# Delta-rule attention in front of two expert stages: scores and changes on the far half of the partitions, outputs as one 128-row matmul per head

## What is computed

```python
# 1: delta rule, for each batch and head
k_n = k / (norm(k) + 1e-06)
for t in range(S):
    y[:, :, t] = q[:, :, t] @ state
    v_old = k_n[:, :, t] @ state
    state = state + beta[t] * outer(k_n[:, :, t], v[:, :, t] - v_old)
# 2: four experts on all tokens, weighted by normalised domain_probs
for e in range(4):
    out += p[:, e:e + 1] * (maximum(x @ w1[e], 0.0) @ w2[e])
# 3: eight experts, each token goes to its best one
logits = normalised(x) @ normalised(emb).T / tau
out[mask_e] = gate[mask_e, None] * (maximum(x[mask_e] @ w1[e], 0.0) @ w2[e])
```

## Time and profile before

| | us |
|---|---|
| median of 3 runs | 1420.02 (1417.57 to 1420.48) |
| the profiled execution | 1416.41 |
| its span | 1414.6 |
| TensorE busy in the span | 1315.2 |
| VectorE, ScalarE, POOL busy | 640.3, 471.1, 625.4 |

### The profile page before, as it was taken

The page is one execution under the profiler, slowest core; times in us unless marked ns, Lnnn a source line. Parts: engine busy times, 40 slices in busy tenths (PEclk is TensorE's granted clock), DMA queues, the critical chain, the costliest instruction groups (busy, mean ns, idle before and its releaser), DMA issues. The chain is left out here.

```text
span 1414.6 us, 31948 instructions
## 1 busy us (share of the span) xinstructions
PE 1315.2 (93%) x13279; PEld 1142.1 (81%) x13280; DVE 640.3 (45%) x1056; ACT 471.1 (33%) x794; POOL 625.4 (44%) x652
## 2 busy tenths in 40 slices
PE   5589999899999999999999999999995599999996
PEld 4468888788888888888788888887784599999996
DVE  7844544354453635437354262223623234636342
ACT  2223223433234422343233433334432213424231
POOL 3382248523684338823487235544652122222221
PEclk9599999999999999999999999999997699999998
DMA  6051233433434243342433323353442224525210
GB/s 237 2 210 58 76 103 103 152 96 65 120 100 172 83 79 109 115 162 72 96 109 97 93 64 84 110 197 108 97 134 75 71 86 129 167 89 172 92 31 23
DMA packets 66401, 149.91 MB, mean 106 GB/s; under 512 B 10676, under 2 KB 26481, under 8 KB 64744
## 3 DMA queue, kind: packets, MB, share of 16 engines
q1 hardware_dynamic: 53512, 116.66, 27.6%
q10 hardware_dynamic: 7776, 20.06, 4.5%
q0 software_dynamic: 4992, 11.44, 2.7%
HBM read 135.85 MB, written 11.48 MB: 104 GB/s over the span
## 5 line engine op out<-in xcount | busy, mean ns | idle before, releaser
L421 POOL TENSOR_TENSOR wsl<-raw,wsh 128x768 fp32r<-128x768 f32 x138 | 253.1, 1835 | 430.1 <-ACT wsh L544 429.8
L783 DVE SCALAR_TENSOR_TENSOR hl<-bank,hh 128x512 fp32r<-128x512 f32 x192 | 132.4, 690 | 498.8 <-ACT hh L548 485.9
L548 ACT ACTIVATE hh<-bank 128x512 fp32r<-128x512 f32 x192 | 114.7, 598 | 584.0 <-PE bank L1176 572.3
L1187 PE MATMUL bank<-hh,wsh 128*128 128x512 f32 x576 | 234.5, 407 | 5.2 <-DVE tmp L813 5.2
L1174 PE MATMUL bank<-xhl,wsh 128*128 128x512 f32 x576 | 225.9, 392 | 6.2 <-DMA xhl<-xhl 4.7
L1188 PE MATMUL bank<-hh,wsl 128*128 128x512 f32 x576 | 226.1, 392 | 0.0
L1189 PE MATMUL bank<-hl,wsh 128*128 128x512 f32 x576 | 225.6, 392 | 0.2 <-issue 0.2
L1175 PE MATMUL bank<-xhl,wsh 128*128 128x512 f32 x576 | 224.9, 390 | 0.0
L1176 PE MATMUL bank<-xhl,wsl 128*128 128x512 f32 x576 | 224.8, 390 | 0.0
L544 ACT ACTIVATE wsh<-raw 128x768 fp32r<-128x768 f32 x192 | 160.7, 838 | 7.8 <-DMA raw<-in_w_soft 7.7
L1174 PEld LDWEIGHTS bank<-xhl,wsh 128*128 128x128 f32 x576 | 108.8, 189 | 30.7 <-issue 4.8
(11 more groups left out here) (206 smaller groups left out, 2134.3 us busy)
## 6 DMA issues: line engine op xcount, KB each, us to landing
raw<-in_w_soft SPq DMA_DIRECT2D x192, 384.0 KB, 3.1
rawT<-in_w_top ACTq DMA_DIRECT2D x48, 384.0 KB, 3.7
kq<-in_kq SPq DMA_DIRECT2D x12, 1024.0 KB, 8.8
pb<-p_scratch SPq DMA_DIRECT2D x24, 256.0 KB, 3.8
rawT<-in_w_top SPq DMA_DIRECT2D x16, 384.0 KB, 6.5
kN<-in_kn SPq DMA_DIRECT2D x6, 768.0 KB, 4.8
vN<-in_vn SPq DMA_DIRECT2D x6, 768.0 KB, 5.4
xs_scratch<-xrow SPq DMA_DIRECT2D x20, 192.0 KB, 3.7
```

Of the source, the lines that this page charges most:

```text
L421: nc.gpsimd.tensor_tensor(wsl[:, n % WB, :], raw[:, n % RB, :], f32(wsh[:, n % WB, :]), ALU.subtract).then_inc(wlp_ok, 1)
L548: nc.scalar.activation(hh[:, n % 2, :], ps_h[n % 2][:, :], ACT.Relu).then_inc(hi_ok, 1)
L783: nc.vector.scalar_tensor_tensor(out=hl[:, n % 2, :], in0=ps_h[n % 2][:, :], scalar=0.0, in1=f32(hh[:, n % 2, :]), op0=ALU.max, op1=ALU.su ...
L1187: nc.tensor.matmul(o, wsh[:, w, cols], hh[:, n % 2, :], start=(f == 0), stop=False)
```

## The change

One tile `QP` now holds, for each head, q features on its own half of the partitions and the masked scores on the other ("far") half. One tile `SU` holds S and U of a head the same way; both are zero in the rows that belong to neither. The output of a head is one matmul over 128 partitions, SU against QP. To get there `scores` and `solved` write to the far half, `deltas` (ScalarE), `masked` and `state` (VectorE) work in two ops, one per head, and kN is stored with its halves exchanged; the squares of k are made from a load of their own, `ks`. q is no longer double-buffered: its two halves are loaded behind the v load. In a scan slot the order on TensorE is now solved, recalled, changes, outputs, the recall of the next step and the change of state of the last one each as a block. `scores` of chunk 0 are masked on VectorE after `back(0)`, no longer by POOL. The sums, norms, system and diagonal of chunk 1 stand behind the states of chunk 0 on VectorE, gram(1) right in front of the loop on TensorE, and the inverse of chunk 1 in slot 1 of POOL's loop. LATE becomes [9, 3, 0, 0, 0, 0].

The diff, cut; left out are the other wide blocks (the same edits as in the scan), renamed arguments and the arrays made on the host.

```diff
-        kq = sb(att, "kq", [P, 2, 2, NPAIR, NCH, HALF])
+        kT = sb(att, "kT", [P, 2, NPAIR, NCH, HALF])
...
-        PT = sb(att, "PT", [P, NU, HALF])
+        QP, SU = sb(att, "QP", [P, 2, NU, HALF]), sb(att, "SU", [P, 2, NPAIR, D])
...
-    ps_ks, ps_u = (bank_s[0][:, AL * D * i:AL * D * i + AL * D].rearrange("p (a d) -> p a d", a=AL) for i in range(2))
+    ps_u, ps_ds = (bank_s[0][:, AL * D * i:AL * D * i + AL * D].rearrange("p (a d) -> p a d", a=AL) for i in range(2))
     ps_yT = bank_s[1][:, 0:256].rearrange("p (a n) -> p a n", a=AL)
-    ps_ds = bank_s[1][:, 256:256 + AL * D].rearrange("p (a d) -> p a d", a=AL)
+    ps_ks = bank_s[1][:, 256:256 + AL * D].rearrange("p (a d) -> p a d", a=AL)
...
-    LATE = [3, 1, 0, 0, 0, 0]
-    INV_SLOT = 18
+    LATE = [9, 3, 0, 0, 0, 0]
+    INV_SLOT, FIRST_INV = 18, 1
     ROUTE = 3
     def att_slot(t, s):
     def inverting(m):
         begun = [SPT * t + INV_SLOT + LATE[t] for t in range(NT - 2)]
-        return m < 6 or any(b <= m < b + 12 for b in begun)
+        return FIRST_INV <= m < FIRST_INV + 12 or any(b <= m < b + 12 for b in begun)
...
+    def load_q(eng, c, hh2):
+        if c:
+            eng.wait_ge(ds_mm, UN * c)
+        eng.dma_start(QP[ROWS_T[hh2], hh2, :, :].rearrange("p u n -> p (u n)"), q_d[c, hh2]).then_inc(q_in, 16)
+
...
         sp.dma_start(en[:, :], emb).then_inc(e_in, 16)
         sp.dma_start(taub[:, 0:1], tau.partition_broadcast(P)).then_inc(e_in, 16)
+        load_squares(0)
+        sp.dma_start(beta[:, :, :], beta_d).then_inc(b_in, 16)
+        load_k(0)
+        load_q(sp, 0, 0)
+        load_v(0)
         load_kn(0)
-        sp.dma_start(beta[:, :, :], beta_d).then_inc(b_in, 16)
-        load_features(0, 0)
-        load_features(0, 1)
-        load_v(0)
-        load_features(1, 0)
-        load_kn(1)
+        load_k(1)
         for n in range(RB):
             load_raw(n)
+        load_squares(1)
+        load_kn(1)
         sp.dma_start(pr[:, :, :], probs_d).then_inc(p_in, 16)
-        load_features(1, 1)
...
         load_v(1)
+        for hh2 in range(2):
+            load_q(sp, 1, hh2)
...
             if s == 1 and t + 2 < NC:
                 load_kn(t + 2)
-                load_features(t + 2, 0)
-                load_features(t + 2, 1)
+                load_k(t + 2)
+                load_squares(t + 2)
             if a == 17 and t + 2 < NC:
                 load_v(t + 2)
+                for hh2 in range(2):
+                    load_q(sp, t + 2, hh2)
...
-        def mask_scores():
-            pool.wait_ge(pc_ok, VN)
-            nc.gpsimd.tensor_tensor(PT[:, :, :], PT[:, :, :], upper[:, :].unsqueeze(1).to_broadcast([P, NU, HALF]),
-                                    ALU.mult).then_inc(p_ok, VN)
-
...
         constants()
-        mask_scores()
         pool.wait_ge(inv_step, INV_STEPS)
         values(0)
         for n in range(2):
             low(n)
-        start_inverse(pool, nc.gpsimd, 1)
-        invert(pool, nc.gpsimd, 1)
-        values(1)
...
+            if n == FIRST_INV:
+                start_inverse(pool, nc.gpsimd, 1)
+                invert(pool, nc.gpsimd, 1)
+                values(1)
...
-            act.wait_ge(kn_in[c % 2], 16 * (c // 2 + 1))
-            if c:
-                act.wait_ge(ssq_ok, 2 * c)
-            nc.scalar.activation(sq[:, :, :], kN[:, c % 2, :, :], ACT.Square).then_inc(sq_ok, 1)
+            act.wait_ge(sq_in, 16 * (c + 1))
+            nc.scalar.activation(sq[:, :, :], sq[:, :, :], ACT.Square).then_inc(sq_ok, 1)
...
             m = UN * c + k
-            if k < UN - 1:
-                act.wait_ge(ks_mm, m + 2)
-            else:
-                act.wait_ge(u_mm, m + 1)
-            if m >= 2:
-                act.wait_ge(ds_mm, m - 1)
-            nc.scalar.activation(U[:, k % 2, :, :], ps_u, ACT.Copy).then_inc(u_ok, 1)
+            act.wait_ge(u_mm, m + 1)
+            act.wait_ge(ch_mm, m)
+            if m >= NB:
+                act.wait_ge(ds_mm, m - NB + 1)
+            pairs = slice(AL * (k % NB), AL * (k % NB) + AL)
+            for hh2, rows in enumerate(ROWS_FAR):
+                last = nc.scalar.activation(SU[rows, hh2, pairs, :], ps_u[rows], ACT.Copy)
+            last.then_inc(u_ok, 1)
         def x_high(c, k):
             ch, b, _ = units_of(k)
             cols = slice(P * b + HALF * ch, P * b + HALF * ch + HALF)
             act.wait_ge(ds_mm, UN * c + k + 1)
+            act.wait_ge(gks_ok, min(UN * c + k + 3, UN * c + UN))
...
+            if v == 0 and c == 0:
+                dve.wait_ge(mask_set, MASKS)
+            scores = score_banks[min(c, 1)][v]
+            for hh2, rows in enumerate(ROWS_FAR):
+                last = nc.vector.tensor_tensor(QP[rows, hh2, eight_pairs(v)[2], :], scores[rows],
+                                               upper[rows].unsqueeze(1).to_broadcast([HALF, 8, HALF]), ALU.mult)
+            last.then_inc(p_ok, 1)
...
             dve.wait_ge(ks_mm, m + 1)
-            if k:
-                dve.wait_ge(u_ok, m)
+            dve.wait_ge(ds_mm, m - 1)
...
-            if m >= NB:
-                dve.wait_ge(s_ok, m - NB + 1)
-            nc.vector.tensor_tensor(S[LIVE, pairs, :], S[LIVE, pairs, :], ps_ds[LIVE, :, :],
-                                    ALU.add).then_inc(s_ok, 1)
+            dve.wait_ge(u_ok, min(m + 2, UN * c + UN))
+            dve.wait_ge(s_ok, m - NB + 1)
+            for hh2, rows in enumerate(ROWS_D):
+                S = SU[rows, hh2, pairs, :]
+                last = nc.vector.tensor_tensor(S, S, ps_ds[rows], ALU.add)
+            last.then_inc(s_ok, 1)
...
         back(0)
-        sums(1)
-        norms(1)
         for v in range(VN):
-            system(1, v)
-        diagonal(1)
+            masked(0, v)
         for i in range(2):
             wide_first_state(i)
...
         for i in range(2):
             wide_state(i)
+        sums(1)
+        norms(1)
+        for v in range(VN):
+            system(1, v)
+        diagonal(1)
         probabilities()
...
-                    k, q = (kq[ROWS_D[hh2], c % 2, i, a0 + a, ch, :] for i in range(2))
-                    last = nc.tensor.matmul(dst[ROWS_T[hh2], a, :], k, q, start=True, stop=True)
+                    k, q = kT[ROWS_D[hh2], c % 2, a0 + a, ch, :], QP[ROWS_D[hh2], hh2, NPAIR * ch + a0 + a, :]
+                    last = nc.tensor.matmul(dst[ROWS_FAR[hh2], a, :], k, q, start=True, stop=True)
             last.then_inc(p_mm, 1)
...
+            pe.wait_ge(u_ok, m)
+            pe.wait_ge(s_ok, m - 1)
+            for al in range(AL):
+                for rows, far in zip(ROWS_T, ROWS_FAR):
+                    last = nc.tensor.matmul(ps_u[far, al, :], TT[rows, units.start + al, :], R[rows, k % 2, al, :],
+                                            start=True, stop=True)
+            last.then_inc(u_mm, 1)
+
+        def recalled_wait(c, k):
+            m = UN * c + k
+            if k == 0:
+                pe.wait_ge(p_ok, VN * (c + 1))
+            pe.wait_ge(s_ok, m - NB + 1)
+            pe.wait_ge(gks_ok, m)
+            pe.wait_ge(xl_ok, m - 2)
+
+        def changes_wait(c, k):
+            m = UN * c + k
+            if k == 0:
+                pe.wait_ge(kn_in[c % 2], 16 * (c // 2 + 1))
+            pe.wait_ge(u_ok, m + 1)
+            pe.wait_ge(xl_ok, m)
+            pe.wait_ge(s_ok, m)
+
+        def recalled(c, k, al):
+            ch, b, _ = units_of(k)
+            pair = AL * b + al
+            for hh2, rows in enumerate(ROWS_D):
+                last = nc.tensor.matmul(ps_ks[ROWS_T[hh2], al, :], kT[rows, c % 2, pair, ch, :], SU[rows, hh2, pair, :],
+                                        start=True, stop=True)
+            if al == AL - 1:
+                last.then_inc(ks_mm, 1)
+
+        def changes(c, k, al):
+            _, b, units = units_of(k)
+            for hh2, rows in enumerate(ROWS_FAR):
+                last = nc.tensor.matmul(ps_ds[ROWS_D[hh2], al, :], kN[rows, c % 2, units.start + al, :],
+                                        SU[rows, hh2, AL * b + al, :], start=True, stop=True)
+            if al == AL - 1:
+                last.then_inc(ch_mm, 1)
+
+        def outputs(c, k):
+            _, b, units = units_of(k)
             for al in range(AL):
                 for hh2 in range(2):
-                    last = nc.tensor.matmul(ps_u[ROWS_T[hh2], al, :], TT[ROWS_T[hh2], units.start + al, :],
-                                            R[ROWS_T[hh2], k % 2, al, :], start=True, stop=True)
-            last.then_inc(u_mm, 1)
-
-        def outputs(c, k):
-            ch, b, units = units_of(k)
-            m = UN * c + k
-            pe.wait_ge(u_ok, m + 1)
-            if m:
-                pe.wait_ge(xl_ok, m)
-                pe.wait_ge(s_ok, m)
-            for al in range(AL):
-                for hh2 in range(2):
-                    nc.tensor.matmul(ps_yT[ROWS_D[hh2], al, :], S[ROWS_D[hh2], AL * b + al, :],
```

(32 more changed lines are left out.)

155 lines of the change are left out of this document (63 added, 92 removed).

## The result

| | kernel before | changed kernel |
|---|---|---|
| median (range), us | 1420.01 (1415.52 to 1428.55), 6 runs | 1441.77 (1434.97 to 1450.48), 6 runs |
| profiled execution, us; its span | 1416.41; 1414.6 | 1434.97; 1433.2 |
| mean granted clock of TensorE | 0.969 | 0.953 |

The ratio is 1.015, 95% interval 1.0105 to 1.0195. The changed kernel is slower by some 22 us; the forecast was 1421.2, range 1411 to 1430. A second build of the same text, run later beside the experiments, gave 1.0176 (1.0159 to 1.0193).

A forecast was written before the change was run, and what follows sets the result against it. TensorE, busy 93% of the span, bounds: small matmuls in the loop, the serial start outside. Terms -14.4 + 5.8 + 9.8 - 5.75 + 5.75 = +1.2 us, on the median 1420.02 giving 1421.2; range 1411 to 1430.

The forecast's parts named there:

- Part 1: Attention slots of the loop: one 128-row output matmul per head saves 0.36 us a slot, -14.4 us (-10 to -18).
- change of shape: TensorE in the slot: one more switch of matmul tile shape takes 0.1 to 0.2 us off the gain.
- Rival D: Outputs in the slot: full-height tiles do not run beside each other; about +21 us, 1441; chance 0.08.
- Part 2: Start, up to the first inverse: -4.2 us; features ready and VectorE's states ended 3.9 us earlier.
- The mask's 4.2 us: Start: without POOL's mask, a VectorE step of chunk 0's inverse no longer takes 4.60 us; 4.2 us off the wait.
- k(0) behind half of q(0): Start: half of q fetched by ScalarE's queue ahead of k costs +0.5 us (0 to 1.3).
- Part 3: Start of the loop: chunk 1's moved VectorE work and load_q(1) make raw(3) 7.3 us late; +5.8 us (2 to 9).
- Part 4: Table LATE, second and third inverse: TensorE waits 8.9 us for TT in slot 37; +9.8 us (7 to 12).
- The wait for tmp: End of tile: the wait with its cold clock leaves tile 0 (-5.75 us) and comes in tile 1 (+5.75).
- Tiles 2 and 3: Loop, slots 65 to 96 and 96 to 128: -2.9 us in each stretch.
- Rival C: Idle stretches cost more than they last, as TensorE comes back cold: +5.9 us, 1426; chance 0.27.
- A new wait shows up in tiles 2 to 5: Profile of the loop's later tiles: a new wait there would make the prediction fall; no size given.

The follow-up runs named there:

- a_order: Changed kernel with changes ahead of recalled in the scan slot (solved, changes, recalled, outputs): 1441.69 us, ratio 1.0191 to the kernel before.
- a_front: Changed kernel with k(0) loaded first, and q(0), v(0) and all that follows only after chunk 0's gram blocks: 1434.10 us, ratio 1.0118 to the kernel before.
- a_q1_late: Changed kernel with the two loads of q(1) issued in slot 5, not in front of raw(3): 1431.26 us, ratio 1.0116 to the kernel before.
- a_probs_first: Changed kernel with the expert probabilities computed on VectorE ahead of chunk 1's sums to diagonals, not behind: 1431.95 us, ratio 1.011 to the kernel before.
- a_best: Changed kernel with probabilities ahead of chunk 1's work, v(1) and q(1) held back, later q in pieces, q(0) and v(0) after chunk 0's gram: 1400.07 us, ratio 0.9922.
- a_pad: Changed kernel with one more SP instruction in slot 4, a wait for a transfer long done: ratio 1.0127 to the kernel before, chip 7.
- a_best_nofront: Changed kernel with probabilities ahead of chunk 1's sums, v(1) and q(1) held back to slots 4 to 8, later q in pieces: 1408.10 us, ratio 0.9982.

## Why the prediction was wrong

Point by point, against the steps of the prediction:

- **Part 1, the slot: right in mechanism, too small.** The forecast was 0.36 us a slot. An undisturbed slot is 0.69 shorter (6.63 to 5.94): 0.25 from blocks that overlap (forecast 0.06; a_order measured it), and the other 0.44 from the outputs, with no loss seen for the change of shape. Rival D (full-height tiles take turns) is refuted: 16 records and the way back take 0.58 us, where turns alone would take 0.91.
- **Part 2, the start: half right.** The mask's 4.2 us came back: TT is there at 47.3, not 48.8, though gram began 2.8 later. The forecast gave 0.5 for k(0) behind half of q(0); it was 2.8 (9.7 to 12.5). With the q halves under way the window from 12 to 14 us moves 168 GB/s at share 0.98, where the kernel before has 402 to 430 at its own gram. a_front, with q(0) held back and k(0) first, starts gram at 7.3.
- **Part 3, the moved work: the step that failed.** It priced q(1) at "1 MB, 2.6 us at 0.40 MB/us", a rate read off a 128-partition transfer. raw(3) was 16.0 us late, and not 7.3: 7.8 for p_set (4.7 forecast; the states end 1.9 later than thought, and chunk 1's work is 1.2 longer, with a wait of 1.0 for its gram), 1.3 for issuing q and 6.9 for q on the way. The two follow each other: a_q1_late, with q(1) out of the way, has raw(3) 7.5 us earlier, and a_probs_first, with p_set early and q(1) still ahead, 10.2 us earlier (8.0 by the time p_scratch is written, the rest behind it). With the cold clock that is +17.7 for +8.9 at slot 3, 9 of the 18 us by which the sum was off.
- **Part 4, LATE: right in each wait, blind behind them.** From slot 36 to 40 the difference rises by 10.0 us; 9.8 was forecast. 6.7 of them are waiting (8.1 forecast). The other 3.3 hold the cold clock (1.65 forecast) less what the kernel before does more of in these slots: TensorE's rows show 0.50 from 292.45 to 301.3, 8.9 us, an estimate of 4.4 us lost. The wait for tmp left tile 0 (-6.0; -5.75 forecast) and came in tile 1 (+5.6; +5.75). Not in the sum were the stalls of slots 45 to 52 (one of 2.3 us at slot 52, which goes with the spread q; 3.1 at slot 46 in the kernel before with LATE alone). In the kernel before, LATE alone costs 17 us, against 6.7 for its terms in the forecast.
- **Tiles 2 and 3: a term that the forecast did not have.** It took -2.9 for each; they came out at +1.2 and +0.9. Without stalls they would stand at -6.1 and -6.3 (a_best). Against that version, slots 81 and 113, with gram under the half-rate q loads, take 3.7 and 1.1 us more, and the scan slots 77, 109 and 110 take 3.6, 2.0 and 4.2 more (the 4.2 in this one profile only; the second build has 2.1, 3.6 and nothing there, and 5.8 and 3.7 in slots 81 and 113).
- **Rival C** said slower because idle stretches cost more. That is so, but with 1426 it gave the wrong size: the extra cold clock of slot 37 is 1.7 to 2.8 of the 18 us.

Of the signs that the prediction listed, the inverse without its 4.6 us step and the wait for tmp in tile 1 instead of tile 0 came as written. The block is 1.64 us and not 2.0, the probabilities start at 85 and not 82, raw(3) is used at 107 and not 98, TensorE is idle for 14.2 us and not 6 ahead of up(3), and it waits 6.7 for TT and not 8 to 9. "A new wait shows up in tiles 2 to 5", which it had named as a condition of its fall, came true.

What stays open is the cause of the stalls of slots 45, 77, 109, 110 and 141 and their exact share in the loss. Slot by slot, against the versions with the later scatter, they cost 14.0 us in the changed kernel and 4.9 in the kernel before, so 9 of the 19.6 us by the ruler; in the second build it is 5 of 22.4. On a chip without them the changed layout should lose less: a_pad, which adds only the idle wait, has 1.0127 on chip 7.

Is the change worth having? On chip 15, where these stalls are missing, a_best is 0.8% faster than the kernel before, 0.9% with interleaving. Part of that is the order of the first loads, which the kernel before could take over as well (not run); without it the layout with its own damage repaired gains 0.2% (a_best_nofront). No repaired version was run on a chip that has the stalls, where they may take some 5 to 9 us of this back (an estimate from the two builds above).

## What to carry to other kernels

Price a transfer by the partitions that it lands on and by what is issued behind it, not by its bytes: here a layout that splits a full-height tile in two halves halved the rate of its load, and the next tile of weights paid. Compare two kernels by a ruler, an op that each repeats in every step: sums of waits hid that the slots had become shorter, and where it was lost. And before a fraction of a per cent is put down to an edit, profile the unedited kernel on the same chip: here a set of stalls was in every profile of three chips and in none of two others, and looked like the work of one idle instruction.
